# A mixing layer and two feed-forward layers: tiles 64 bytes lower, the first chunk's tail mixed in two banks, the second chunk's main channels split sooner

## The reference

```python
w = softmax(weight)                  # (8 heads, 7 taps)
x = causal_depthwise_mix(x, w)       # out[s, c] = sum_k w[head(c), k] * x[s - 6 + k, c]; x is (2, 4096, 192)
x = (silu(x @ w_gate) * (x @ w_val)) @ w_out       # 192 -> 1536 -> 192
h = x @ w_in
out = elu(h) @ w_out2                              # 192 -> 2048 -> 192
```

## Time and profile before

| | us |
|---|---|
| median of 3 runs (lowest, highest) | 1193.2 (1192.63, 1193.23) |
| the profiled execution's own time | 1191.55 |
| its span, first to last instruction | 1189.7 |
| PE busy | 1184.1 |
| DVE, POOL, ACT busy | 772.7, 699.6, 664.6 |

### The profile page before, as it was taken

One profiled execution on the slowest core, in us unless ns is written; L12 is line 12 of the kernel. 1 busy time (PEld: TensorE's weight loads), 2 busy tenths in 40 slices (PEclk: granted clock), 3 DMA queues, 4 the chain that ended last, 5 costly groups with the idle time before them and its releaser, 6 DMA issues.

```text
span 1189.7 us, 31406 instructions
## 1 busy us (share of the span) xinstructions
PE 1184.1 (100%) x11804; PEld 1051.1 (88%) x11804; DVE 772.7 (65%) x1192; ACT 664.6 (56%) x1113; POOL 699.6 (59%) x517
## 2 busy tenths in 40 slices
PE   9999999999999999999999999999999999999998
PEld 8889889898898988989888898888989889898898
DVE  7877565675656766566665766647667475675665
ACT  6557455464654646546465564655646555465564
POOL 6378565474654746547465474654756556475565
PEclk9999999999999999999999999999999999999999
DMA  8512011121101211012110021100212002120110
GB/s 179 121 43 45 18 31 32 31 44 31 24 20 31 44 31 26 18 31 44 31 35 17 22 44 31 35 18 22 44 31 44 9 22 44 31 44 9 32 33 15
DMA packets 103957, 43.38 MB, mean 36 GB/s; under 512 B 75889, under 2 KB 93937, under 8 KB 103921
## 3 DMA queue, kind: packets, MB, share of 16 engines
q1 hardware_dynamic: 103104, 42.29, 16.5%
q10 hardware_dynamic: 816, 0.59, 0.2%
HBM read 16.12 MB, written 6.29 MB: 19 GB/s over the span
## 4 chain that ended last, share of the span: by engine, by line
PE 97%; DVE 2%; issue 1%; ACT 0%; DMA 0%; SPq 0%; DVEq 0%; ACTq 0%
PE up L897 54%; PE down L897 42%; DVE hid_lo L740 1%; DVE mixed L702 1%; DVE hidden L759 0%; DMA in_b_lo<-in_b_lo 0%; DVE x_t L720 0%; DVE in_b_lo L708 0%; ACT act L568 0%; PE down L1108 0%; ACT out_w L324 0%; ACT hidden L641 0%; ACT in_b_hi L526 0%; ACT in_a_hi L646 0%; SPq L370 0%
## 5 line engine op out<-in xcount | busy, mean ns | idle before, releaser
L448 POOL TENSOR_TENSOR hid_lo<-hidden,hid_hi 128x512 fp32r<-128x512 f32 x435 | 607.1, 1407 | 464.6 <-ACT hid_hi L585 302.2
L897 PE MATMUL down<-out_w,hid_hi 64*128 64x384 f32 x2040 | 300.8, 355 | 0.0
L759 DVE TENSOR_TENSOR hidden<-act,up 128x512 f32<-128x512 f32 x191 | 131.0, 686 | 242.4 <-ACT act L568 242.4
L897 PE MATMUL down<-out_w,hid_lo 64*128 64x192 f32 x2040 | 263.0, 247 | 0.0
L800 DVE TENSOR_SCALAR act<-up 128x512 f32<-128x512 f32 x256 | 164.8, 686 | 107.5 <-PE up L897 105.4
L897 PE MATMUL up<-in_b_hi,up_w_hi 64*128 64x512 f32 x1128 | 226.1, 391 | 0.2 <-DMA in_b_lo<-in_b_lo 0.2
L897 PE MATMUL up<-in_b_lo,up_w_hi 64*128 64x512 f32 x1128 | 225.2, 389 | 0.0
L897 PE MATMUL up<-in_b_hi,up_w_lo 64*128 64x512 f32 x1128 | 224.5, 388 | 0.0
L585 ACT ACTIVATE hid_hi<-hidden 128x512 fp32r<-128x512 f32 x192 | 121.5, 633 | 174.9 <-DVE hidden L759 156.5
L621 ACT ACTIVATE hid_hi<-hidden 128x512 fp32r<-128x512 f32 x256 | 156.7, 628 | 96.8 <-DVE hidden L816 79.9
L897 PEld LDWEIGHTS down<-out_w,hid_lo 64*128 64x128 f32 x2040 | 202.1, 187 | 4.5
(11 more groups left out here) (99 smaller groups left out, 1100.6 us busy)
## 6 DMA issues: line engine op xcount, KB each, us to landing
x_raw<-x_dram SPq DMA_DIRECT2D x136, 64.0 KB, 2.3
out_dram<-stage SPq DMA_DIRECT2D x15, 384.0 KB, 2.7
in_b_hi<-in_b_hi SPq DMA_DIRECT2D x32, 128.0 KB, 2.3
in_b_lo<-in_b_lo SPq DMA_DIRECT2D x32, 128.0 KB, 2.3
swapped<-halves SPq DMA_DIRECT2D x32, 128.0 KB, 2.3
in_a_hi<-in_a_hi SPq DMA_DIRECT2D x30, 128.0 KB, 2.3
in_a_lo<-in_a_lo SPq DMA_DIRECT2D x30, 128.0 KB, 2.3
stage<-w_out_dram SPq DMA_DIRECT2D x7, 384.0 KB, 4.4
```

The source lines that it names most:

```text
L448: return pool.tensor_tensor(hid_lo[:, slot, :], hidden[:, s, :], hid_hi[:, slot, :].bitcast(F32), ALU.subtract)
L759: v.tensor_tensor(hidden[:, f % 2, :], act[:, f % 2, :], val_bank(f, n)[:, :], ALU.mult)\
L897: return nc.tensor.matmul(dst, lhsT, rhs, start=start, stop=stop, skip_group_check=True)
```

## The change

- `WIDE` goes from 120 to 104: the two matmuls that spread the taps have 104 columns, and every tile behind `taps_head` starts 64 bytes lower, 128 bytes above a multiple of 2048 for the inputs and hidden tiles.
- The second half of chunk 0's tail is mixed into `MIX1 = down[1]`, and `mix0_ready` is given after each half. ACT makes the high part of slot TWICE in two halves of 256 tokens, and DVE the low part in two halves. Five low parts are counted in place of four.
- ACT splits two pieces of weights before them, not three; the third follows after CROSSED.
- `first_blocks` takes the products in the outer loop: high by high of blocks 0 and 1, low weights of both, low data of both.
- Chunk 1: ACT makes MAIN's high part once mixing step 13 is done (not all 16), TWICE's once step 14 is done; DVE makes MAIN's low part before `chunk0_lo(9)`.

```diff
-    WIDE = 120
+    WIDE = 104
+        MIX1 = down[1]
-        FIRST_PARTS = 4
+        FIRST_PARTS = 5
+        FIRST_MADE = {TWICE: 2, MAIN: 3, CROSSED: FIRST_PARTS}
-        BEFORE0 = 3
+        BEFORE0 = 2
...
                 if part == 0:
-                    a.wait_ge(mix_step, mixed_before(c + 1))
+                    a.wait_ge(mix_step, mixed_before(c) + MIX - 2 if is_int(c, 1) else mixed_before(c + 1))
                     if not is_int(c, 1):
                         a.wait_ge(val_ready, N1 * c)
+                elif is_int(c, 1):
+                    a.wait_ge(mix_step, mixed_before(c) + MIX - 1)
...
-            a.wait_ge(mix0_ready, 1)
-            nc.scalar.activation(in_a["hi"][:, TWICE, :], MIX0[:, :], ACT.Copy).then_inc(first_hi, 1)
+            for half, bank in enumerate((MIX0, MIX1)):
+                t = slice(half * T // 2, (half + 1) * T // 2)
+                a.wait_ge(mix0_ready, half + 1)
+                nc.scalar.activation(in_a["hi"][:, TWICE, t], bank[:, t], ACT.Copy).then_inc(first_hi, 1)
...
                     if f == 9 and is_int(n, 0):
+                        input1_lo(1, 0)
                         chunk0_lo(9)
-                        input1_lo(1, 0)
                         input1_lo(1, 1)
...
-            first_input_lo(TWICE, MIX0[:, :], 1)
+            first_input_lo(TWICE, MIX0, 1, slice(0, T // 2))
+            first_input_lo(TWICE, MIX1, 2, slice(T // 2, T))
...
             def first_blocks():
+                for slot in (TWICE, MAIN, CROSSED):
+                    turned = (1, 0, 2)[slot]
+                    for wpart, part in (("hi", "hi"), ("lo", "hi"), ("hi", "lo")):
+                        for f in (0, 1):
+                            if slot == TWICE and part == "hi":
+                                wait_weights(pe, UP1_AT[f])
+                            pe.wait_ge(first_hi if part == "hi" else first_lo, FIRST_MADE[slot])
+                            c = slice(f * P, (f + 1) * P)
+                            a, z = slot == TWICE and wpart == part, slot == CROSSED and part == "lo"
+                            gate = mm(gate_bank(f)[:, :], up1_w[wpart][TOP, slot, c], in_a[part][TOP, slot, :], a, z)
+                            val = mm(val_bank(f)[:, :], up1_w[wpart][LOW, turned, c], in_a[part][LOW, slot, :], a, z)
...
                     if half == 0:
                         pe.wait_ge(diag_done, k + 1)
-                    last = mm(MIX0[:, t0:t1], diag[:, k, :], paired[:, 2 * k + t0:2 * k + t1], k == 0, k == PAIRS - 1)
-            last.then_inc(mix0_ready, 1)
+                    elif k == 0:
+                        pe.wait_ge(tap_step, TAP_STEPS)
+                    last = mm((MIX0, MIX1)[half][:, t0:t1], diag[:, k, :], paired[:, 2 * k + t0:2 * k + t1],
+                              k == 0, k == PAIRS - 1)
+                last.then_inc(mix0_ready, 1)
```

More of the change, by code:

```diff
@@ L294, in mix_ffn_ffn @@
                 OUT2_AT[at * OT] = len(pieces)
-        AHEAD, READY, FIRST_PIECES = 6, 5, 2
+        AHEAD, READY = 6, 5
         BESIDE0 = {2: 5, 3: 6, 5: 7, 7: 8, 8: 9}
@@ L499, in _ @@
             for i in range(READY):
-                if i == FIRST_PIECES:
+                if i == BEFORE0:
                     pool.wait_ge(first_lo, FIRST_PARTS)
@@ L861, in _, with first_input_lo @@
                     v.scalar_tensor_tensor(dst, src, tap0, dst, ALU.mult, ALU.add).then_inc(mix_step, 1)
-            def first_input_lo(slot, full, made):
+            def first_input_lo(slot, full, made, t=slice(0, T)):
                 v.wait_ge(first_hi, made)
-                v.tensor_tensor(in_a["lo"][:, slot, :], full, in_a["hi"][:, slot, :].bitcast(F32), ALU.subtract)\
+                v.tensor_tensor(in_a["lo"][:, slot, t], full[:, t], in_a["hi"][:, slot, t].bitcast(F32), ALU.subtract)\
                     .then_inc(first_lo, 1)
             def first_crossed_lo(to, of):
-                v.wait_ge(first_hi, 2)
+                v.wait_ge(first_hi, FIRST_MADE[MAIN])
                 v.tensor_tensor(in_a["lo"][to, CROSSED, :], mixed[of, 0, :], in_a["hi"][of, MAIN, :].bitcast(F32),
                                 ALU.subtract).then_inc(first_lo, 1)
-            first_input_lo(TWICE, MIX0[:, :], 1)
+            first_input_lo(TWICE, MIX0, 1, slice(0, T // 2))
+            first_input_lo(TWICE, MIX1, 2, slice(T // 2, T))
             for part, turned_x in enumerate((X_MAIN, X_TAIL)):
                 v.tensor_copy(halos[:, 1, part, :], turned_x[:, T - HALO:T]).then_inc(mix_step, 1)
-            first_input_lo(MAIN, mixed[:, 0, :], 2)
+            first_input_lo(MAIN, mixed[:, 0, :], FIRST_MADE[MAIN])
             first_crossed_lo(TOP, LOW)
@@ L919, in first_blocks @@
             def first_blocks():
[L920 to L930, removed]
+                for slot in (TWICE, MAIN, CROSSED):
[9 more added lines that the diff above has]
+                            val = mm(val_bank(f)[:, :], up1_w[wpart][LOW, turned, c], in_a[part][LOW, slot, :], a, z)
+                            if z:
+                                gate.then_inc(gate_ready, 1)
+                                val.then_inc(val_ready, 1)
             def both(upper, lower, w, data, start, stop):
```

## The result

The changed kernel takes 1181.38 us, median of 6 runs (1179.64 to 1182.18), against 1193.22 (1192.63 to 1193.55, 6 runs): a ratio of 0.990, 95% interval 0.9888 to 0.9913. The forecast was 1192.6 with a range down to 1190.2, so the time lies 8.8 us outside it. What was forecast is there too, but it is at most a tenth of the gain.

A forecast was written before the change was run, and what follows sets the result against it. PE, busy 1184.1 of 1189.7 us, was taken as the bound. About 0.6 us saved at the start, 0 per pair, took the profiled 1191.55 to 1190.9; plus 1.65 for the runs' median, 1192.6 (range 1190.2 to 1194.4).

The forecast's parts named there:

- the 64 bytes: Tiles behind the taps tile lie 64 bytes lower; claimed to change PE's rate by 0 per pair.
- rival B: PE's pairs run faster at the new addresses, each ns per pair 5.9 us; 1 ns gives 1187; chance 11%.
- The 12 ns between the forms: Mixing matmuls at about 217 ns against pairs at 229; 12 ns x 3,840 pairs = 46 us, the most to be won.
- Rival C: PE's pairs run slower at the new addresses; by 2 ns per pair, 12 us, giving 1204; chance 5%.
- The start: PE up to chunk 1's first input: first pair at 11.26, block 2 at 15.45, crossing at 49.07; 0.63 us gained in all.
- The order of products: First two blocks: four pairs ahead of the first needing low data, so no gap before it; covered by 0.10 us.
- DVE's half low parts: DVE's two half subtractions for chunk 0's low part, taken at 0.43 us each, between 0.35 and 0.69.
- The narrower tap matmuls: Four tap matmuls at PE's start, 104 columns for 120: between 0 and 0.13 us shorter, taken as 0.05.
- ACT's delay: Three casts on ACT make block 0's Silu start at 15.58, 0.15 late; block 3 gets its bank at 17.65, due 17.51.
- the 0.33: Gain left at block 3: it started at 17.98 and would get its bank from DVE at 17.65.
- the early split: Chunk 1's input chain 0.78 us sooner by its own steps, 0.15 later by ACT; PE released at 49.07, before 49.70.
- Rival D: PE's full clock rate comes only behind the 16 mixing matmuls: 3.5 us more, 1196; chance 4%.

The follow-up runs named there:

- m2_scan: TensorE's pairs alone, no layers, 24 per group, data start moved against the weights in 16-byte steps, then halves and narrower shapes; 226.7 ns at 0, 233.8 at 32.
- e3_behind32: Changed kernel with 32 bytes of padding in front of x_raw, so data and hidden tiles lie at distance 32 from the weights; 1205.04 us (1 run).
- e5_behind128: Changed kernel with 128 bytes of padding in front of x_raw, so data and hidden tiles lie at distance 128 from the weights; 1204.16 us (1 run).
- e8_old_order: Changed kernel with the products of the first two blocks in the old order, the halves in two banks kept; 1179.78 us (single time).
- e2_before104: Kernel before with one edit, WIDE 104 for 120; 1182.42 us, ratio 0.9909.
- e1_wide120: Changed kernel with WIDE back at 120, so tiles behind the taps tile lie 64 bytes higher as before; 1192.51 us, ratio 0.9994 to the kernel before.

## Why the prediction was wrong, step by step

**The step that failed** is the one on the 64 bytes: "I take 0 per pair." It measured some 2.2 ns for each of 3,840 pairs of 512 columns (228.9 to 226.7) and some 1.2 ns for each pair of the second down projection ((2.27 - 2.25) / 16), 10.7 us in all. The mechanism had been named, as rival B, with 11%, "each ns per pair is 5.9 us": by it 2 ns on nearly all pairs, 11 to 12 us, is what came. Two of my reasons against it don't hold. First, "nothing in the trace shows a rate that follows an address" was true and worth nothing: in this trace the quantity never varies. The weights start at the same remainder of 256 in every column block, and so do all slots of the inputs and hidden tiles, so all pairs of 512 columns had the distance 64. An even rate over rows that all share a value is no evidence that the value doesn't count. Second, the mixing matmuls "as even as any" at starts 8 bytes apart are float32 matmuls of 256 columns. No run here moves that form, and the fp32r pairs of 256 columns in m2_scan show no slow distance either (120 ns at 0, 118 at 32, 64 and 128), so an even rate there says nothing of 512 columns. It is not that they take whole rows: those have the step too, at 512 columns. The 12 ns between the forms, which I gave as the most to be won, are not on offer: 226.7 is the best of all distances tried.

**Rival C** (slower by addresses) was the same mechanism: 32 or 128 bytes cost 11.9 and 10.8 us over the kernel before, as e3_behind32 and e5_behind128 show, close to the 12 us at which it was priced. The sign hung on the two remainders, and the description of the kernel before had both, 128 and 192.

**The start** was right in its mechanisms. From the first mixing matmul to the first pair: 4.48 us before, 4.25 in e8_old_order, which had the same early rate; 0.23, where 0.21 (with the tap matmuls outside, 0.26 less 0.05) was forecast. The order of products: 0.24, forecast 4.40 - 4.19 = 0.21. DVE's half low parts cost 0.41 and 0.42 us (0.43 taken). The narrower tap matmuls, taken at 0.05, gave 0.04, 0.24 and 0.30 in the three executions with 104 columns and the early rate (e3_behind32, e2_before104, e8_old_order: 4.92, 4.72 and 4.66 against 4.96). They follow the moment of the full rate, which lies within these matmuls: the clock's record starts at 4.67, 4.27 and 4.13 us there, and at 4.74 in the kernel before. What is next late there was not foreseen: at the early rate PE's first pair in e8_old_order is released by POOL's low part of the second weight piece, as its row says.

**ACT's delay** was the step of the start that failed. ACT does run three casts without a gap and Silu right behind them, but block 3 starts 18.98 - 16.94 = 2.04 us after block 2, nine pairs at 226.7, without a stall. ACT's rows in the changed kernel:

```profile
15.93 0.83 ACT L326 ACTIVATE up_w_hi<-stage 128x768 fp32r<-128x768 f32 x1
16.91 0.60 ACT L572 ACTIVATE act<-up 128x512 f32<-128x512 f32 x1
```

The casts end at 16.76 and Silu starts at 16.91, 0.15 later. PE was late in this execution, but e3_behind32, with the early rate and its first pair at 11.25, has no stall either:

```profile
14.72 0.83 ACT L327 ACTIVATE up_w_hi<-stage 128x768 fp32r<-128x768 f32 x1
15.49 1.09 ACT L573 ACTIVATE act<-up 128x512 f32<-128x512 f32 x2
```

```profile
16.12 1.29 DVE L766 TENSOR_TENSOR hidden<-act,up 128x512 f32<-128x512 f32 x2 [2.06 <-ACT act L573]
```

There the casts do hold Silu back, but by 0.06 (15.49 against 15.43 before) and not 0.15, and DVE's two multiplications end at 16.12 + 1.29 = 17.41, where the forecast had 17.59; block 3 starts at 17.62, nine pairs behind block 2 at 15.53. So the 0.33 that this was to leave, and the 0.29 after it, were not the limit, and the early split came to its full 0.56. By parts the start gives 0.23 + 0.24 + 0.56 = 1.0 us, where 0.63 was forecast. By the timed runs it is 0.6 (e1_wide120 beside the kernel before, an interval that includes none and 1.8) to 1.0 (e2_before104 less the changed kernel, medians taken on different occasions).

**Rival D**, the full rate that comes late, is in the profiled execution: its first pair is at 12.73 where the forecast without it was 11.26 and e3_behind32 had 11.25. It costs about 1.5 us there. It is not the narrower tap matmuls: e1_wide120 has them 120 wide and its 16 mixing matmuls take 4.68 us, while e2_before104, e3_behind32 and e8_old_order have 104 and 3.69. The record of the granted clock starts at 4.13 to 4.74 us in the four early executions and at 8.87 to 10.42 us in the eight late ones. Both modes occur with the new start, as the spread of the six runs (1179.64 to 1182.18) is in keeping with. Whether the new start makes the late one more frequent (8 of its 10 profiled executions, none of the 2 with the old start) isn't settled. The timed runs speak against it: the two early executions with the old start are 1.65 us (1191.55) and 1.6 us (1180.85) below the medians of their kernels, about what the late rate costs, so most runs of the old start may be late ones too. The 1.65 us that the forecast put on top of the profiled time would then be this. The runs without a trace can't show it. The Trainium skill's "TensorE: Matmul & The Clock Gate", Part 1, says that the point of release does not follow the kernel's start and so varies from run to run. Executions of one and the same program weren't profiled twice here, so it is not shown.

**What stays open**: which two reads collide. The facts are that one half's stream slows with the distance of its own weights, by 256 bytes; that the lower half decides in a pair, though the upper alone slows as much when it runs alone; that the alternating groups decide for neither load; that pairs stay uneven for up to ten pairs behind a slow stretch; and that steps of 16 bytes depend on the tile too. The Trainium skill's "SBUF — State Buffer", "SBUF: two separate sides", says that the matmul's data and LDWEIGHTS have independent read ports and that PE waits for no one. The group of m2_scan at distance 0 against the one at 32, 226.7 and 233.8 ns with every other engine idle, does not fit the reading that the two never disturb each other.

## What to carry to other kernels

When an engine is busy all the time and a change moves its operands, an even rate in the trace of before proves nothing: ask first whether any two rows differ in the quantity that is moved, and if none do, keep both signs in the range, at a small step of its pace times the number of instructions: here 2 ns times 5,900 pairs, 12 us, which the forecast had worked out and left out of its range. For fp32r matmuls of 512 columns, in 64-row pairs or with whole rows, start the data at the same remainder of 256 bytes as the weights; 64 bytes off costs a pair 1% and 32 or 128 bytes off 3% (1% and 2% of this kernel's time). When a rate is read from a group of instructions, leave out the first ones: the run-in and the switch between forms hid the step of the whole rows in an average over 18. Padding tiles in front of one group at a time (the weights too, the other engines' tiles, the inputs alone) separates place, distance and owner in four runs.

## What the runs showed of the hardware

- A pair of 64-row matmuls of 512 fp32r columns starts, once run in, every 226.7 ns with data and weights at the same remainder of 256 bytes, every 228.3 to 229.6 at 64 bytes, and every 232.5 to 233.9 at the other multiples of 32 (averages over a group, with the granted clock at 1.00). One half alone costs as much as the pair. Whole-row matmuls have the same pace once run in: 226.7 to 227 at 0, 229 at 64, 233.7 at 32, 232.6 at 128.
- Behind a slow group, pairs at distance 0 or 256 need up to ten pairs to come down to 226.7 ns; that is some 0.04 us each time. A switch between pairs and whole rows costs some 0.2 us (two starts 0.33 to 0.34 us apart in place of 0.23). At 256 and 192 columns the distance changed nothing beyond 1 to 2 ns, at 384 nothing that followed it.
- Busy ACT, DVE and POOL beside the pairs changed their pace by nothing that shows (4.08, 4.21 and 4.12 us for 18 pairs with them, 4.08, 4.21 and 4.11 without).
- TensorE's first matmuls run at about half pace, and the full pace came either by 5 us (eight 128-column turning matmuls in 1.09 us; the clock's record starts at 4.13 to 4.74 us) or only after 8 us (in 1.97 us; at 8.87 to 10.42). The views read 1.00 in both, also ahead of that record. It moves the start of the first pair by 1.5 to 2.2 us (12.71 to 13.47 against 11.25).
